# Attention and two feed-forward blocks on one core: four of SyncE's loads change places in a hand-written slot table

## The reference, cut to what matters

```python
# 1. attention: coarse (means of 4 neighbours) plus local (|i - j| < 4)
q_d, k_d, v_d = (t.reshape(B, H, S // 4, 4, D).mean(axis=3) for t in (q, k, v))
out_up = np.repeat(softmax(scale * q_d @ k_d.T) @ v_d, 4, axis=2)
out_local = softmax(where(mask, scale * q @ k.T, -1e9)) @ v
x = out_up + out_local
# 2. layer norm, 512 -> 2048 -> 512 with relu, and the residual
x = x + relu(norm(x) * g_ln @ w_ch1) @ w_ch2
# 3. mix with the position before, 512 -> 1024 -> 512 with relu squared, gated
y = sigmoid(xr @ w_r) * (relu(xk @ w_k) ** 2 @ w_v)
```

## Time and profile before

| | us |
|---|---|
| median of 3 runs | 768.27 (767.16 to 768.62) |
| profiled execution, its own device time | 768.22 |
| span of the profiled execution | 766.0 |
| PE busy | 751.8 (98% of the span) |
| DVE, ACT, POOL busy | 431.0, 272.6, 232.3 |
| mean granted clock of PE | 0.989 of full speed |

### The profile page before, as it was taken

How to read it: one execution, slowest core, us unless ns; L and a number is a source line. 1 busy time by engine, 2 the same in 40 slices (tenths; PEclk the granted TensorE clock), 3 DMA queues, 4 the chain that set the end, 5 groups by cost and what they waited for, 6 DMA issues and landing times.

```text
span 766.0 us, 15806 instructions
## 1 busy us (share of the span) xinstructions
PE 751.8 (98%) x6433; PEld 693.8 (91%) x6433; DVE 431.0 (56%) x805; ACT 272.6 (36%) x620; POOL 232.3 (30%) x268
## 2 busy tenths in 40 slices
PE   7799999999999999999999999999999999999998
PEld 6699999999999999999999999998888888888886
DVE  5676764444654354554354332567686676766655
ACT  3665423223233223233233231546334434333322
POOL 5666753132444223345223222004111111111101
PEclk9699999999999999999999999999999999999999
DMA  9992451220440121341011003612003011010010
GB/s 188 236 288 59 80 116 18 47 60 11 89 109 20 29 41 55 65 99 40 14 26 39 15 2 138 231 56 87 0 1 110 0 52 33 0 56 1 0 56 28
DMA packets 116543, 49.67 MB, mean 65 GB/s; under 512 B 95084, under 2 KB 105592, under 8 KB 116472
## 3 DMA queue, kind: packets, MB, share of 16 engines
q1 hardware_dynamic: 116472, 48.68, 24.8%
HBM read 39.20 MB, written 9.45 MB: 64 GB/s over the span
## 4 chain that ended last, share of the span: by engine, by line
PE 93%; SPq 2%; DVE 2%; DMA 1%; POOL 1%; issue 1%; ACT 0%; DVEq 0%; ACTq 0%
PE psH L1081 26%; PE psY L1098 25%; PE psH L1132 13%; PE psY L1153 13%; PE psA L1114 6%; PE psA L978 2%; PE psA L1009 2%; PE psA L954 1%; PE psA L914 1%; SPq L597 1%; PE psA L989 1%; PE psA L927 1%; DMA k_first<-in_k_dram 1%; SPq L585 1%; DMA v_raw<-in_v_dram 1%
## 5 line engine op out<-in xcount | busy, mean ns | idle before, releaser
L1081 PE MATMUL psH<-xc_hi,w_hi 128*128 128x288 f32 x512 | 156.0, 305 | 2.6 <-DVE xc_lo L1596 2.6
L1098 PE MATMUL psY<-h_hi,w_hi 128*128 128x288 f32 x512 | 153.2, 299 | 0.3 <-DVE y_tmp L1643 0.2
L1081 PE MATMUL psH<-xc_lo,w_hi 128*128 128x288 f32 x512 | 152.0, 297 | 0.0
L1081 PE MATMUL psH<-xc_hi,w_lo 128*128 128x288 f32 x512 | 151.9, 297 | 0.0
L1098 PE MATMUL psY<-h_lo,w_hi 128*128 128x288 f32 x512 | 150.8, 294 | 0.0
L1098 PE MATMUL psY<-h_hi,w_lo 128*128 128x288 f32 x512 | 150.7, 294 | 0.0
L1741 DVE SCALAR_TENSOR_TENSOR h_lo<-psH,h_hi 128x288 fp32r<-128x288 f32 x128 | 58.3, 456 | 164.0 <-ACT h_hi L1437 163.6
L1437 ACT ACTIVATE h_hi<-psH 128x288 fp32r<-128x288 f32 x128 | 52.5, 410 | 247.1 <-PE psH L1081 246.4
L883 POOL TENSOR_TENSOR relu_k<-relu_k 128x512 f32<-128x512 f32 (+1 forms) x39 | 38.6, 990 | 243.8 <-ACT relu_k L1392 243.8
L1081 PEld LDWEIGHTS psH<-xc_hi,w_hi 128*128 128x128 f32 x512 | 97.0, 190 | 5.3 <-issue 4.1
L1098 PEld LDWEIGHTS psY<-h_hi,w_hi 128*128 128x128 f32 x512 | 96.1, 188 | 2.5 <-issue 1.3
(11 more groups left out here) (189 smaller groups left out, 1343.7 us busy)
## 6 DMA issues: line engine op xcount, KB each, us to landing
w_raw<-in_moe_w_ch_dram SPq DMA_DIRECT2D x8, 1024.0 KB, 8.7
v_win<-in_v_dram SPq DMA_DIRECT2D x84, 56.0 KB
x_scratch<-x SPq DMA_DIRECT2D x8, 576.0 KB, 4.2
out_dram<-gate SPq DMA_DIRECT2D x17, 256.0 KB, 2.2
raw<-in_q_dram SPq DMA_DIRECT2D x112, 36.0 KB, 2.0
raw<-in_k_dram SPq DMA_DIRECT2D x96, 36.0 KB, 1.9
v_raw<-in_v_dram SPq DMA_DIRECT2D x12, 288.0 KB
x_sh<-x_scratch SPq DMA_DIRECT2D x3, 1026.0 KB, 5.6
```

What stands on the lines that cost most here:

```text
L1081: ins = mm(psH[:, m % 2, 0:N], ws[a][:, kt, f * P:(f + 1) * P], xx[bb][:, kt], start=(kt == 0 and i == 0), stop=(kt == KT - 1 and i == 2))
L1098: ins = mm(psY[:, d, 0:N], ws[a][:, f, d * P:(d + 1) * P], hs[bb][:, m % 2], start=(f == 0 and i == 0), stop=(f == NF1 - 1 and i == 2))
```

## The change

Two edits are made. A new number `AV_LOAD = 4` is subtracted where SP looks up the AV steps, so that each window load of the frames stands four slots later in SP's program: slot 19 in place of 15, and 25 in place of 21 (21 and 27 in frame 0). In frame 0 alone, the load of the third part of the value sums stands in slot 23 in place of 25, and POOL's sum of the second part in slot 22 in place of 24.

```diff
@@ -89,6 +89,8 @@
     ROOT_OUT, ROOT_IN = 3, 10
     BEHIND = 2
+
+    AV_LOAD = 4
@@ -165,7 +167,7 @@
     for b in range(1, B):
         behind = BEHIND if b == 1 else 0
-        for g, (s, load) in enumerate(((16 + behind, 8), (22 + behind, 17 + behind), (28 + behind, 21 + 2 * behind), (39, 31))):
+        for g, (s, load) in enumerate(((16 + behind, 8), (22, 17 + behind), (28 + behind, 21 + behind), (39, 31))):
             V_SUM[SLOTS * (2 * b - 2) + s] = (b, g)
             V_LOAD[SLOTS * (2 * b - 2) + load] = (b, g)
@@ -691,7 +693,7 @@
                 if slot in V_LOAD:
                     load_v_sum(*V_LOAD[slot])
-                for kind, u, n in steps_at(slot):
+                for kind, u, n in steps_at(slot - AV_LOAD):
                     for part in parts_of(kind, u, n):
                         if kind == "AV" and NW_U * u + part + 2 < NWIN:
                             load_window(NW_U * u + part + 2)
```

## The result

| | before | changed |
|---|---|---|
| median | 767.76 us (4 runs) | 787.42 us (787.21 to 788.11, 4 runs) |
| ratio | | 1.0257, 95% interval 1.0239 to 1.0275 |
| span of the profiled execution | 766.0 us | 786.0 us |
| mean granted clock of PE | 0.989 | 0.978 |

The change made the kernel 2.6% slower. The sign and the waits were forecast; the forecast counted two falls of PE's clock and three came. Runs of one kernel differ by 1 to 2 us with PE's mean clock (of 23 runs of the kernel before, 17 have 0.989 or less and a median of 767.79 us, 6 have 0.995 or more and a median of 766.5), so that 0.1% between two kernels can be one of how many runs of each kind they drew.

The account below looks back on a forecast made before the run. PE, busy 98% of the span, was taken as the bound. Waits of 14.0 us, less 0.8 for the early third load, plus 3.6 for two clock falls, gave 16.8 us on 768.22: 785.0 us, range 779.4 to 790.2.

Parts of the forecast that it names:

- the scenario that came, three: Rival: PE's clock falls in all three waits at the full price of 2.35 us each, 788.5 us; chance 0.16.
- PE pays every wait in full: In the frames PE is always busy, so any wait is lost whole, with no idle time later to catch up.
- Waits of 3.5, 5.1 and 5.4 us, 14.0 in all: At the second AV step of frames 0, 2 and 4 PE waits for window 3u+2, bounds 12.2 to 15.5 us.
- Odd frames and second pairs at nothing: Frames 1, 3, 5 unchanged; each unit's other two windows (3u+3, 3u+4) are read over 35 us later, so cost nothing.
- The early third load gives 0.8 us: Value sums, frame 0: the earlier third load removes PE's wait for what follows POOL's sum, a gain of 0.47 to 1.0 us.
- Two falls of the clock at 1.8 us, 3.6 in all: Behind the waits PE's clock drops to half speed twice, 1.8 us each; chance 0.42.
- The upper bound of 2.35 for one fall: High end of a fall's cost, from 4.7 us of work at half speed after the restart at 36.06 us.
- the row at 23 us: The earlier trace's one clock fall, 1.00 to 0.50 by 24 us, taken to agree in kind with the skill page.
- The window in time: Rival: the window lands in time and the early third load alone decides, 767.4 us, faster by 0.1%; chance 0.02.
- The clock holds: Rival: the waits come but PE's clock holds, 781.4 us, or falls once, 783.2 us; chance of none or one 0.36.
- That the shift does less than it says: Rival: SP, blocked by its waits, is late in any order, so the slot shift matters less; no chance of its own.

Follow-up runs that it names:

- the second pairs alone: Changed kernel, but only the loads of windows 3u+3 and 3u+4 stand four slots later, that of window 3u+2 where it was: 767.40 us, ratio 0.9997.
- the one-frame kernel: Changed kernel, but of the windows 3u+2 only window 11, that of frame 2, is loaded four slots later: 774.47 us, ratio 1.0084.

## Why the prediction was right, step by step

The direction, the path and the three waits were right. The clock was not: the forecast had two falls, and the scenario that came, three, had been given 0.16. The time still fell into the range, since its high end had been drawn at three falls.

- **PE pays every wait in full.** Right. The four stretches of the ledger sum to the span's difference with nothing made up later.
- **Waits of 3.5, 5.1 and 5.4 us, 14.0 in all.** Measured 3.77, 5.43 and 4.79, 14.0 in all. That the sums agree is luck, for two errors of opposite sign cancel. The time from the last issue to PE's start was taken as 1.3 us from the earlier trace rows, where nothing else was in flight, and was 2.0, 2.3 and 1.8 (85.15 to 87.16, 210.29 to 212.57, 339.31 to 341.15): 2.2 us too little in all. The issues were put too late against the reader, by 0.4, 0.6 and 1.5 us: in frame 0 the window took 1.82, not 2.17; in frames 2 and 4 the second eight pieces of q took 3.87 and 3.88, not half of 8.53 and of 9.11; in frame 4 the window took 1.82, not 2.52. And the 5.4 of frame 4 had been chosen between 5.1 and 5.8.
- **Odd frames and second pairs at nothing.** Right: no wait there, and 767.40 us with the second pairs alone. In frame 1 of the changed kernel the first AV step ends at 135.96 and SP issues the window at 136.02, as was said.
- **The early third load gives 0.8 us.** The size was right (0.73 in the trace of the kernel with that edit alone), the attribution wrong: with frame 0's wait ahead, PE's wait for `y_tmp` goes away without that edit.
- **Two falls of the clock at 1.8 us, 3.6 in all.** This is the term that was too small, in the count and in the size. There were three falls. Taking the waits out of the ledger, and adding the 0.73 of the start of frame 1, leaves 1.52, 2.48 and 2.94 us, 6.9 in all. The upper bound of 2.35 for one fall was no bound: it was read off the only fall of the trace, and the low stretch after the restart was 4.7 us there and 5.5 and 6.7 us in frames 2 and 4. By these measured terms the sum is 14.0 + 6.9 - 0.7 = 20.2; the ledger's first row, where PE reached the step 0.2 us sooner, brings it to the 20.0 measured.
- **What the page and the row at 23 us bear.** The Trainium skill, page "TensorE: Matmul & The Clock Gate", section "HAM oscillation — how this bites in real kernels", says that a wait on a DMA of some microseconds puts TensorE back to half clock, so that the matmuls behind it start cold. This case agrees: in the traces of the changed kernel and of four others all 13 waits of 3.6 to 5.4 us brought a fall. The row at 23 us, which the prediction took to agree in kind, does not bear on it: PE's gaps ahead of that fall were 0.50 and 0.41 us long and ended with POOL, not with a DMA. What brought that fall stays open.
- **The rivals.** The window in time: false. The clock holds: false in the traces of the changed kernel and of the four with a wait of 3.6 us or more and PE idle; true at 2.0 us or less in the two profiled executions that have it. That the shift does less than it says: false in frames 0, 2 and 4, where the window is issued behind the pieces that it was moved behind. It is true that from three slots to four nothing changes, since no DMA stands between.

## What to carry to other kernels

A load in a queue that issues in order is late by what stands ahead of it, not by the number of slots: add up the issues, the waits among them and the landing, and compare with the reader's time. Where the bounding engine has no slack, each such wait costs its own length, and in these traces a PE wait of 3.6 to 5.4 us cost another 1.5 to 2.9 us, since the clock is low behind it. When two edits are timed together, a wait that one of them brings can cover the wait that the other was to remove, and then the gain of the second is not there to be had.

## What the runs showed of the hardware that had not been expected

- From the end of the issue of the same four DMAs of 56 KB to PE's start it is 1.7 to 2.3 us with pieces of q or k in flight, and 2.7 to 2.8 us directly behind a load of 288 KB. With nothing else under way the transfer ended 1.2 us after the issue.
- A fall of the clock can begin after the wait: in frame 0 PE started again at 87.16 and the clock fell at 88.4. Of the 13 falls, ten began while PE still stood, and the clock was low for 6.8 us each time; three began 0.2 to 1.3 us after PE had started again, and it was low for 3.4 us. No run tests what decides between the two.
- The length of the wait does not set the cost of a fall; the part of the low stretch in which PE works does. The fall cost 1.5 us for 3.4 us of work at half clock (changed kernel, frame 0), 1.9 for 4.4 (the one-frame kernel), 2.5 for 5.5, 2.9 for 6.6 (`AV_LOAD = 3`, frame 0) and 2.9 for 6.7 us: some 0.44 us for each microsecond, and 0.43 to 0.50 in all 13 falls.
